# Attention scores of two heads as 64-row products, five rounds to a pair, in a fused attention and MoE kernel

## The reference

```python
batch, n_heads, seq, head_dim = (4, 8, 1152, 64)
q_pool = q.reshape(B, H, S // factor, factor, D).mean(axis=3)      # factor = 2
scores = scale * np.matmul(q_pool, k.transpose(0, 1, 3, 2))
scores = scores - np.max(scores, axis=-1, keepdims=True)
attn = np.exp(scores)
attn = attn / (np.sum(attn, axis=-1, keepdims=True) + 1e-09)
return np.matmul(attn, v).astype(np.float32)
```

## Time and profile before

| what | value |
|---|---|
| median of 3 runs | 930.46 us (929.25 to 930.73) |
| profiled execution, its own time | 927.38 us |
| profiled execution, span of the trace | 925.5 us |
| PE busy | 859.7 us (93%) |
| PEld busy | 624.4 us (67%) |
| DVE busy | 559.0 us (60%) |
| ACT busy | 474.4 us (51%) |
| POOL busy | 432.6 us (47%) |

### The profile page before, as it was taken

The page is one execution under the profiler, slowest core; times in us unless marked ns, Lnnn a source line. Parts: engine busy times, 40 slices in busy tenths (PEclk is TensorE's granted clock), DMA queues, the critical chain, the costliest instruction groups (busy, mean ns, idle before and its releaser), DMA issues. The chain is left out here.

```text
span 925.5 us, 16088 instructions
## 1 busy us (share of the span) xinstructions
PE 859.7 (93%) x5498; PEld 624.4 (67%) x5498; DVE 559.0 (60%) x1167; ACT 474.4 (51%) x686; POOL 432.6 (47%) x277
## 2 busy tenths in 40 slices
PE   4899999999999999999999999878769999999998
PEld 4676676776666767766766766554225888888886
DVE  4676676676676666766666766450007676666763
ACT  4455455555555555555554554321009666666662
POOL 2845746746647548449448440000008644433343
PEclk9999999999999999999999999989979999999999
DMA  5443303203203113023033043706991000000000
GB/s 133 154 112 81 80 2 80 71 8 79 51 28 79 29 50 79 10 69 79 0 79 80 1 156 144 268 6 248 395 401 46 24 24 23 23 23 23 23 18 27
DMA packets 84208, 76.53 MB, mean 83 GB/s; under 512 B 42448, under 2 KB 62928, under 8 KB 83664
## 3 DMA queue, kind: packets, MB, share of 16 engines
q1 hardware_dynamic: 81840, 75.52, 26.0%
q10 hardware_dynamic: 2336, 0.59, 0.3%
HBM read 71.37 MB, written 4.72 MB: 82 GB/s over the span
## 5 line engine op out<-in xcount | busy, mean ns | idle before, releaser
L608 ACT ACTIVATE prob<-ps,neg_max 128x1152 f32<-128x1152 f32 x144 | 175.4, 1218 | 74.1 <-DVE spare L558 74.1
L371 PE MATMUL ps<-ident,prob 128*128 128x128 f32 x1296 | 202.8, 284 | 10.5 <-ACT prob L608 8.0
L553 DVE TENSOR_REDUCE part_neg<-ps 128x1 f32<-128x512 f32 x288 | 186.0, 683 | 25.1 <-PE ps L355 24.8
L371 PEld LDWEIGHTS ps<-ident,prob 128*128 128x128 f32 x1296 | 144.4, 141 | 82.8 <-issue 36.6
L471 DVE COPY probT<-ps 128x512 f32<-128x512 f32 (+1 forms) x256 | 124.5, 487 | 121.5 <-PE ps L371 109.7
L355 PE MATMUL ps<-kT,qT_hi 128*128 128x512 f32 (+1 forms) x480 | 176.7, 386 | 3.8 <-issue 3.1
L619 ACT ACTIVATE probT<-ps 128x512 f32<-128x512 f32 x144 | 86.1, 598 | 159.4 <-PE ps L371 157.6
L388 PE MATMUL ps<-probT,v_nat 128*64 128x256 f32 (+1 forms) x1152 | 163.8, 415 | 1.1 <-DVE probT L469 1.0
L355 PE MATMUL ps<-kT,qT_lo 128*128 128x512 f32 (+1 forms) x480 | 159.7, 356 | 0.0
L224 POOL TENSOR_TENSOR qT_hi<-q_raw,ones 64x576 fp32r<-64x576 f32 x60 | 68.5, 1142 | 168.3 <-PE ps L355 144.2
L355 PEld LDWEIGHTS ps<-kT,qT_hi 128*128 128x128 f32 x480 | 94.4, 202 | 20.4 <-issue 10.1
(11 more groups left out here) (145 smaller groups left out, 1051.5 us busy)
## 6 DMA issues: line engine op xcount, KB each, us to landing
slot<-in_moe_w SPq DMA_DIRECT2D x16, 2048.0 KB, 12.6
v_nat<-in_v SPq DMA_DIRECT2D x16, 576.0 KB, 4.8
k_nat<-in_k SPq DMA_DIRECT2D x30, 288.0 KB, 4.1
q_nat<-in_q SPq DMA_DIRECT2D x32, 256.0 KB, 4.3
out<-res SPq DMA_DIRECT2D x18, 256.0 KB, 2.0
slot<-in_moe_w_in SPq DMA_DIRECT2D x2, 2048.0 KB, 20.6
slot<-in_moe_w_out SPq DMA_DIRECT2D x8, 512.0 KB, 16.7
q_nat_r<-in_q SPq DMA_DIRECT2D x32, 64.0 KB, 3.8
```

Source lines behind the costliest of these rows:

```text
L371: last = nc.tensor.transpose(block_at(s, kt), src[:, kt * P:(kt + 1) * P], ident[:])
L553: nc.vector.tensor_reduce(part[:, c:c + 1], slot_banks(s)[:, c, :], AX.X, ALU.min).then_inc(part_done, 1)
L608: nc.scalar.activation(prob[prob_index(par, n)][:], slot_row(s), ACT.Exp, bias=neg_max[:, n:n + 1], scale=-1.0, accum_out=sums).then_inc(e ...
```

## The change

Two tiles, the same query tile of both heads, now make one round, and the mixed tile a round of its own: five rounds for a pair, in the order 0, 1, mixed, 2, 3. K's high part of both heads stands in one tensor of 128 partitions (head 0 above, head 1 below), its low part in another, and the same holds for Q. A tile takes three products of 64 rows for each chunk (high Q with high K, high Q with low K, low Q with high K; that of the two low parts is left out), and the products of head 0 (rows 0 to 63) and of head 1 (rows 64 to 127) are issued in turn, into different banks. That makes 81 products for a pair: 72 of 64 rows in four rounds, and 9 of 128 rows in the mixed one.

Head 0's scores have banks 0 to 2 and head 1's banks 3 to 5. The turned probabilities go back into banks of the same round, so the scores of a round start when those of the round before have been copied out. K (L234) and Q are turned in the mixed round; VectorE, not ScalarE, copies K out of PSUM; POOL splits in four instructions of 128 partitions. `PV_AT` says where the products with V stand: before or between the turns of the two heads. The diff, cut to its core:

```diff
-    SEQ = [('T', 0), ('T', 1), ('Q', 0), ('T', 2), ('T', 3), ('T', 4), ('K', 0), ('T', 5), ('E', 0), ('T', 6), ('T', 7), ('T', 8)]
+    ROUND = (0, 1, None, 2, 3)
+    ROUNDS = len(ROUND)
+    MIX = ROUND.index(None)
-    PV_STEPS = [{8: (0, 6), 10: (6, 14), 12: (14, 18)}, {14: (0, 2), 15: (2, 10), 18: (10, 14), 19: (14, 18)}]
+    PV_AT = {(3, 0): (0, 0, 0, 8), (3, 1): (0, 0, 8, 10), (4, 0): (0, 0, 10, 18),
+             (0, 0): (1, 1, 0, 10), (0, 1): (1, 1, 10, 12), (1, 0): (1, 1, 12, 18)}
+    OUT_AT = {1: 0, 3: 1}
+    PV_EVAC_AT = {0: 0, 2: 1}
...
+            def split_high_low(n, par):
+                pool.wait_ge(k_copied, n)
...
+                pool.tensor_tensor(kT[par][:, 0, :], k_raw[:], ones[:].broadcast_to([P, S]), ALU.mult).then_inc(k_high, 1)
+                pool.wait_ge(k_high, n)
+                pool.tensor_tensor(kT[par][:, 1, :], k_raw[:], kT[par][:, 0, :].bitcast(F32), ALU.subtract).then_inc(k_low, 1)
...
+            def scores(p, par, r, c):
+                k0, k1 = CHUNK[c][0] * P, CHUNK[c][1] * P
+                t = ROUND[r]
+                at = slice(0, P) if t is None else slice((t + 1) * P, (t + 2) * P)
+                for n, (q, part) in enumerate(((qT_hi, 0), (qT_hi, 1), (qT_lo, 0))):
+                    if t is None:
+                        last = nc.tensor.matmul(ps[:, c, 0:k1 - k0], q[par][:, at], kT[par][:, part, k0:k1], start=(n == 0), stop=(n == 2))
+                        continue
+                    for h in range(2):
+                        last = nc.tensor.matmul(ps[:, 3 * h + c, 0:k1 - k0], q[par][HALF[h], at], kT[par][HALF[h], part, k0:k1],
+                                                start=(n == 0), stop=(n == 2))
+                last.then_inc(scores_full, 1)
...
+            def body(p, par, first, last):
+                for r in range(ROUNDS):
+                    for c in range(NCH):
+                        banks_free(p, r, c, first, last)
...
+                        scores(p, par, r, c)
+                    wait(pe, first_evac, tiles_of(p, r))
+                    if r == MIX and not last:
+                        wait(pe, second_b, doubles_of(p, r))
+                        turn_q_rest(p + 1, ps[:, TBANK - 1, BANK - P:BANK])
+                        turn_k_and_q(p + 1, q_row)
+                    if r in OUT_AT and not first:
+                        turn_out(p - 1, OUT_AT[r])
+                    visit(p, par, r, 0, first)
+                    turn_prob(p, r, 0)
+                    visit(p, par, r, 1, first)
+                    if r != MIX:
+                        if r in OUT_AT and not first:
+                            pe.wait_ge(out_evac, (p - 1) * 2 + OUT_AT[r] + 1)
+                        turn_prob(p, r, 1)
...
+            def banks_free(p, r, c, first, last):
+                before = tiles_of(p, r)
+                if c == 0:
+                    wait(pe, first_evac, before - (0 if r == MIX + 1 else 1))
+                    if r == MIX + 1 and not last:
+                        pe.wait_ge(k_copied, p + 1)
+                elif c == 1:
+                    wait(pe, second_a, p * ROUNDS + r)
+                    wait(pe, third_evac, before)
+                elif r == MIX + 1 and not last:
+                    pe.wait_ge(q_evac, p + 1)
+                elif r != MIX:
+                    wait(pe, second_b, doubles_of(p, r))
```

More of the change, by code:

```diff
@@ L122, in over_pairs @@
             body(PAIRS - 1, 1, False, True)
[L124 to L153, removed]
         block = ctx.enter_context(nc.Block())
@@ L374, in pv, with turn_prob @@
+            def turn_prob(p, r, h):
+                tau = tiles_of(p, r) + h
+                pe.wait_ge(exp_done, tau + 1)
+                for c in range(NCH):
+                    dst = turned(h, c)
+                    for n, kt in enumerate(range(*CHUNK[c])):
+                        last = nc.tensor.transpose(dst[:, n * P:(n + 1) * P], prob[h][:, kt * P:(kt + 1) * P], ident[:])
+                    last.then_inc(ptr_full, 1)
             def pv(p, par, g, lo, hi):
-                if lo == hi:
-                    return
@@ L449, in body @@
-                            wait(pe, k_low, p * 2)
-                            wait(pe, q_low, p * 4)
-                        fill(0)
-                        fill(1)
-                    if tile2:
-                        prob_chunk(p - back, par ^ back, j, s, 2, None)
-                    if job:
-                        fill(2)
-                    for g, b, (lo, hi) in groups_at(s, PV_STEPS, first, last):
-                        pv(p - b, par ^ b, g, lo, hi)
+                                pe.wait_ge(first_ql, 1)
@@ new lines, in body @@
+            def body(p, par, first, last):
+                for r in range(ROUNDS):
+                    tau = tiles_of(p, r)
+                    for h in range(heads_of(r)):
+                        maximum(p, r, h)
+                    if r == 0 and not first:
+                        invert(p - 1, par ^ 1)
+                    if r in OUT_AT and not first:
+                        result(p - 1, OUT_AT[r])
+                    if r == MIX and not last:
+                        dve.wait_ge(ktr_full, p + 2)
+                        wait(dve, k_low, p)
+                        nc.vector.tensor_copy(k_raw[:], k_row).then_inc(k_copied, 1)
+                    group_free(dve, p, r)
+                    dve.wait_ge(ptr_full, tau * NCH + 2)
+                    evac(nc.vector.tensor_copy, r, 0, 1).then_inc(second_a, 1)
+                    dve.wait_ge(ptr_full, tau * NCH + 3)
+                    evac(nc.vector.tensor_copy, r, 0, 2).then_inc(third_evac, 1)
+                    if r != MIX:
+                        dve.wait_ge(ptr_full, tau * NCH + NCH + 3)
+                        evac(nc.vector.tensor_copy, r, 1, 2).then_inc(third_evac, 1)
+                if last:
+                    invert(p, par)
+                    result(p, 0)
+                    result(p, 1)
@@ new lines, in empty_v @@
+            def empty_v(p, g):
+                act.wait_ge(pv_done, p * 2 + g + 1)
+                wait(act, otr_full, p * 2 + g - 1)
+                copy(outT[g][:], ps[:, VBANK, 0:GN[g]]).then_inc(pv_evac, 1)
+            def body(p, par, first, last):
+                for r in range(ROUNDS):
+                    tau = tiles_of(p, r)
+                    if r in PV_EVAC_AT and not first:
+                        empty_v(p - 1, PV_EVAC_AT[r])
+                    for h in range(heads_of(r)):
+                        exponential(p, par, r, h)
+                    group_free(act, p, r)
+                    act.wait_ge(ptr_full, tau * NCH + 1)
+                    evac(copy, r, 0, 0).then_inc(first_evac, 1)
+                    if r == MIX:
+                        if not last:
+                            act.wait_ge(qtr_full, p + 2)
+                            act.wait_ge(k_copied, p + 1)
+                            wait(act, q_low, p)
+                            nc.scalar.activation(q_raw[:], q_row, ACT.Copy, scale=EXP_SCALE).then_inc(q_evac, 1)
+                    else:
+                        act.wait_ge(ptr_full, tau * NCH + NCH + 1)
+                        evac(copy, r, 1, 0).then_inc(first_evac, 1)
+                        act.wait_ge(ptr_full, tau * NCH + NCH + 2)
+                        evac(copy, r, 1, 1).then_inc(second_b, 1)
+                if last:
+                    empty_v(p, 0)
+                    empty_v(p, 1)
```

471 lines of the change are left out of this document (144 added, 327 removed).

## The result

| what | before | after |
|---|---|---|
| median of 4 runs each | 929.86 us (928.15 to 930.73) | 918.09 us (917.29 to 918.97) |
| ratio, 95% interval | | 0.9876 (0.9856 to 0.9895) |
| profiled execution, its own time | 927.38 us | 917.36 us |
| last division of the attention ends | 593.54 us | 584.06 us |

The changed kernel is 1.2% faster, 11.8 us by the medians where 17.7 were forecast. The time lies in the forecast's range (898 to 935) and in the likeliest case's own (905 to 921). Between the two profiled executions it is 10.0 us. Of these 9.5 are there when the attention ends; the rest of the program takes 331.5 us, and 332.0 before.

What follows compares the result with a forecast made beforehand. TensorE bounds the kernel before; after the change a chain across engines sets each round. 14.65 + 16 x 34.33 + 4.5 + 7.4 = 575.8 us against 593.54, 17.7 less, so 930.46 - 17.7 = 912.8 us, range 898 to 935.

Steps and rivals of the forecast that it cites:

- likeliest case: Whole kernel: the forecast as computed, give or take 0.12 us a round, 905 to 921 us; chance 0.58.
- Overlap: Scores on TensorE: the two heads' 64-row products run at the same time, a pair of products each 0.23 us.
- rival 2: Scores on TensorE: no overlap, products 0.23 us apart, a round 8.45, a pair 40.5, total 1011 us; chance 0.07.
- rival 1: Scores on TensorE: row groups overlap only in part; at 0.30 us a pair of products, 932 us; chance 0.12.
- The chain sets the round: Each round: its time comes from a chain across engines, not TensorE's sum; 34.33 us a pair against 35.60.
- rival 4: Handoffs between engines cost more than the rows say; 0.28 us more in each of 64 rounds eats all; chance 0.08.
- The exponential starts 0.45 after it: Chain of a round: ScalarE's exponential starts 0.45 us after VectorE's joining instruction, at 2.98 for head 0.
- joining one 1.32 later: Chain of a round: head 1's joining instruction on VectorE starts 1.32 us after its minima start, at 4.19.
- The ninth turn starts 0.87 after the first, and 64-row scores 0.20 after that: End of a round on TensorE: from head 1's first turn at 6.00 to the next round's scores at 7.07 us.
- Two to three rounds: Start of the attention: two to three rounds run at half rate, 9.3 us each, 4.5 us more in all.
- POOL and the split of K and Q: POOL's twelve instructions become four, at most 10.6 us, with 15.4 us left until the next pair; costs nothing.
- Rival 3: The clock falls as TensorE idles; a slow round costs 2.2 us, a quarter of the rounds makes 948 us; chance 0.05.

Runs made afterwards that it cites:

- e8_one_row_group: The changed kernel with both heads' scores products on the same 64 rows, so head 1 gets head 0's scores: 1022.22 us, ratio 1.0964.
- e2_late_wait_last: The changed kernel with the late wait placed last ahead of the joining minimum and the exponential, long-fulfilled waits before it: 911.48 us, ratio 0.9814 to the kernel before.
- e4_one_minimum: The changed kernel with head 1's two minima and join replaced by one minimum over its three banks: 903.60 us, ratio 0.9743 to the kernel before.
- e5_rebalanced: The changed kernel with products with V only before head 0's turns and the second group's turn back in the mixed round: 915.25 us, ratio 0.9852.
- e1: The changed kernel with head 0's three scores products of a chunk issued first, then head 1's: 923.68 us, ratio 0.9952 to the kernel before.
- e3: The changed kernel without every second K tile of the products with V (10 of 18 remain): 918.54 us, ratio 0.9894 to the kernel before.

## Why the prediction was right, and where it was off

- **Overlap.** Right in full. A pair of products every 0.23 us, head against head 3 ns apart; e8_one_row_group confirms rival 2's chain (a pair 40.85, worked out 40.5). The Trainium skill, "TensorE: Matmul & The Clock Gate", section on the measured speedup against the span model, has four row groups at 3.07 times; with two row groups the traces have 0.79 us against 1.49 for six products, 1.9 times, and 0.23 against 0.46 for two behind the burst's first interval, 2.0 times. So rival 1, whose 0.30 us an interval came near that page, did not happen. The 0.01 us that the forecast added to an interval for the second weight load is not there either: the intervals are the 0.23 of the earlier trace rows.
- **The chain sets the round.** Right. With 8 of 18 products with V gone a pair is 0.14 us shorter, and each edit of the chain moves the time. In round 3 TensorE's products with V set it, as forecast: e2_late_wait_last and e4_one_minimum leave it at 7.63, e5_rebalanced brings it to 7.37.
- **The chain's terms.** Here the forecast was off; this is rival 4 in part, handoffs that cost more. The step "The exponential starts 0.45 after it" is 0.53 in the loop, and head 1's "joining one 1.32 later" with its 0.34 before, 1.66, is 1.76. Both were the shortest intervals of before: of its 144 joins 12 start 1.32 behind the first minimum, and most 1.39 to 1.43. Counted over its trace from 60 to 500 us, 38 of 111 exponentials start 0.45 or 0.46 behind their join and the other 73 later, most of them 0.56 to 0.68; one row had been taken for the rule. In the changed kernel the commonest is 0.53. In the mixed round it is 0.61, which is all of that round's excess over the forecast. In round 1 of the loop e2_late_wait_last brings both intervals back to the forecast's numbers; it saves 0.88 us a pair. The step "The ninth turn starts 0.87 after the first, and 64-row scores 0.20 after that" is 1.14, not 1.07: the first interval of a burst is longer, as the prediction itself had said of scores and not of turns.
- **Round by round**, forecast and measured: 7.12 and 7.33; 7.03 and 7.15; 5.68 and 5.84; 7.38 and 7.63; 7.12 and 7.11. The last was right by luck, by two errors that cancel: a join 0.15 earlier (2.43 after the start, where 2.53 and the 0.05 for weight loads were forecast) and the rest 0.15 longer. The sum is 0.73 more than 34.33. With the written-out pairs, which are nearer to the forecast (34.69), it is 10.0 us over the 15 pairs behind the first.
- **Round 3 is the longest.** Right: eight products with V of 320 columns delay head 0's turns to 322.06, 4.67 after the round's start at 317.39.

```profile
318.18 0.33 PEld L254 LDWEIGHTS ps<-kT,qT_hi 64*128 64x128 f32 x4 [0.26 <-DVE probT L361]
...
319.75 2.38 PE L296 MATMUL ps<-probT,v_nat 128*64 128x320 f32 x16
...
322.06 1.20 PE L280 MATMUL ps<-ident,prob 128*128 128x128 f32 x9
```

The first row is a wait of this round alone, for VectorE's copy of the mixed round, which the prediction had foreseen as the one place for it.
- **The start.** Off the other way. "Two to three rounds" at half rate, 4.5 us more: in the profiled execution only the first round is (9.48 us, then 7.03), and the first pair takes 37.20 us where 38.83 were forecast. In the profiles of four of the other kernels (e1, e2, e3, e5) the second round is slow too, 8.70 to 8.93 us, so the forecast's two rounds do happen, but not in every execution. The first scores start at 14.64 (forecast 14.65).
- **The end.** 7.3 us against 7.4, and the products with V in it take 4.11 us as in the earlier trace rows.
- **The balance.** +10.0 from the pairs, -1.6 from the start and -0.1 from the end make 584.1 of the forecast's 575.8; measured 584.06. So the start made the forecast look better than its chain was.
- **POOL and the split of K and Q.** Costed at nothing. POOL's busy time falls from 432.6 to 248.7 us, and it waits for VectorE's copy of K for 72.6 of 100 us. Right.
- **Rival 3, the clock.** The granted clock is 1.00 in 300 to 400 us although TensorE waits 9 us of 100. It didn't happen in the loop; it does at both ends, for some executions.

## What to carry to other kernels

When a change makes one engine's work shorter but puts the steps of a tile one behind another with nothing between them, add up the chain with every handoff before the engine's sum, take the handoffs from rows where the waiting instruction is of the same kind, and look for what is cheap to shorten in it. Where waits take register values, the wait that ends last stands last, next to the instruction; where they are constants the same order cost 0.06 us here. Two small edits that each seem to give little can each be what hides the other: try them together, here 1.95 us a pair for 0.86 and 0.29.

## What the runs showed of the hardware

- Products in two row groups ran alongside each other although the program lists them one group after the other: three products of head 0 stand ahead of head 1's first, and the trace has the starts of the two heads 10 ns apart. The Trainium skill, "TensorE: Matmul & The Clock Gate", section on the mechanism of packing, says that matmuls keep the program's order in start and end. The trace of e1_heads_in_sequence disagrees for the starts across row groups; that the ends keep it no run here shows.
- Weight loads of 64 rows run in parallel as well: the four of a burst's first products take 0.30 us from first start to last end, and 0.76 in e8_one_row_group.
- A register instruction that waits between an event and the instruction behind it costs 0.11 us on VectorE and 0.08 on ScalarE.
- Two 64-row products in two row groups take the 0.23 us of one 128-row product; nothing is lost to their two results going to two banks at once, which the prediction had held possible.
